# One core, three fused transformer stages: the same steps in another order in three written-out lists

## The reference, cut to what matters

```
# 1: attention, 8 heads of 64; heads 0-3 local (32 keys back), heads 4-7 strided (same position mod 32)
x = softmax(masked(q @ k.T / 8)) @ v
# 2: mixing
theta = x @ w_theta
zr, zi = x * cos(theta), x * sin(theta)
u = x + w_tok_r @ zr + w_tok_i @ zi          # over tokens
x = u + relu(u @ w_ch)
# 3: four attention experts with causal softmax; each token takes the best 2 of 4 gates
logits = x @ w_gate; w = softmax(top 2 of logits)
for e in range(4):
    q, k, v = x @ wq[e], x @ wk[e], x @ wv[e]
    out += gate[e] * (causal_softmax(q @ k.T / 8) @ v @ wo[e])
```

## Time and profile before

| | |
|---|---|
| median of 3 runs | 561.27 us (560.54 to 561.74) |
| the profiled execution, its time | 561.68 us |
| its span | 559.9 us |
| busy: PE, DVE, ACT, POOL | 538.1, 320.1, 236.9, 109.5 us |
| mean granted clock of TensorE | 0.994 |
| share of the chain that ended last: PE, DVE, ACT, POOL | 80%, 7%, 2%, 1% |

### The profile page before, as it was taken

How to read it: one execution, slowest core, us unless ns; L and a number is a source line. 1 busy time by engine, 2 the same in 40 slices (tenths; PEclk the granted TensorE clock), 3 DMA queues, 4 the chain that set the end, 5 groups by cost and what they waited for, 6 DMA issues and landing times.

```text
span 559.9 us, 13648 instructions
## 1 busy us (share of the span) xinstructions
PE 538.1 (96%) x5593; PEld 455.5 (81%) x5593; DVE 320.1 (57%) x795; ACT 236.9 (42%) x599; POOL 109.5 (20%) x123
## 2 busy tenths in 40 slices
...
GB/s 214 177 174 26 52 39 189 136 61 28 2 2 2 37 49 125 88 45 45 2 2 2 19 67 75 96 83 31 21 1 0 20 67 1 1 2 1 1 1 85
DMA packets 79997, 28.97 MB, mean 52 GB/s; under 512 B 75200, under 2 KB 75200, under 8 KB 79936
## 3 DMA queue, kind: packets, MB, share of 16 engines
...
## 4 chain that ended last, share of the span: by engine, by line
PE 80%; DVE 7%; SPq 5%; ACT 2%; issue 2%; DMA 1%; POOL 1%; POOLq 0%; DVEq 0%; ACTq 0%
PE acc L1227 41%; PE wide L1227 16%; PE wide L1326 4%; PE turned L1419 3%; PE turned L1360 2%; SPq L604 2%; PE turned L1461 2%; DVE nmax L982 2%; PE turned L1346 2%; PE turned L1395 2%; PE wide L1380 2%; PE wide L1305 2%; PE turned L1260 1%; DMA raw_v<-in_v 1%; SPq L607 1%
## 5 line engine op out<-in xcount | busy, mean ns | idle before, releaser
L769 POOL TENSOR_TENSOR xu_lo<-xt,xu_hi 128x576 fp32r<-128x576 f32 x15 | 21.0, 1411 | 207.3 <-ACT xu_hi L861 207.3
L759 POOL TENSOR_TENSOR probs<-probs,weight 128x128 f32<-128x128 f32 (+4 forms) x36 | 26.9, 767 | 156.9 <-DVE weight L1036 156.9
L839 ACT ACTIVATE probs<-wide,nmax 128x128 f32<-128x128 f32 (+4 forms) x72 | 39.2, 554 | 36.0 <-DVE nmax L982 35.8
L834 ACT ACTIVATE tiled<-wide,nmax 128x64 f32<-128x64 f32 x176 | 39.2, 330 | 24.0 <-DVE nmax L978 20.2
L1227 PE MATMUL wide<-w_tok_hi,z_hi 128*128 128x288 f32 x216 | 47.5, 301 | 0.0
L1227 PE MATMUL wide<-w_tok_lo,z_hi 128*128 128x288 f32 x216 | 46.3, 295 | 0.0
L1227 PE MATMUL wide<-w_tok_hi,z_lo 128*128 128x288 f32 x216 | 46.3, 295 | 0.0
L850 ACT ACTIVATE pt<-turned 128x384 f32<-128x384 f32 (+1 forms) x32 | 16.5, 516 | 56.5 <-PE turned L1360 56.5
L1227 PE MATMUL acc<-xu_hi,w_ch_hi 128*128 128x288 f32 x128 | 39.3, 307 | 1.0 <-DVE xu_lo L1125 0.9
L1227 PE MATMUL acc<-x_hi,w_qk_hi 128*128 128x288 f32 x128 | 39.7, 310 | 0.0
L982 DVE TENSOR_REDUCE nmax<-wide 128x1 f32<-128x128 f32 (+4 forms) x72 | 33.9, 512 | 8.2 <-PE wide L1331 8.1
...
## 6 DMA issues: line engine op xcount, KB each, us to landing
...
```

Of the source, the lines that this page charges most:

```text
L759: ins = g.tensor_tensor(pr, pr, weight[:, j:j + 1].broadcast_to([P, n]), ALU.mult)
L769: g.tensor_tensor(xu[1][:, p, :], xt[:, p, :], xu[0][:, p, :].bitcast(F32), ALU.subtract)\
L834: e = a.activation(tiled[:, t, hh * W:(hh + 1) * W], wide[slot][:, at0:at0 + W], ACT.Exp, bias=nmax[:, hh, t:t + 1])
L839: e = a.activation(probs[:, hh, to0:to0 + n], wide[slot][:, at0:at0 + n], ACT.Exp, bias=nmax[:, hh, j:j + 1], accum_out=sums[:, hh, j:j + 1])
```

## The change

The steps of the three lists are the same, each as often as before. Their order differs in all three; no other line of the kernel is changed. Cut to the places named later ("-" before, "+" after):

```diff
 PROLOGUE = [
-    ("tail", "s1", 2, 0, 2), ("piece", 0), ("back", "s1", 0, 0), ("turn", "s1", 1, 0), ("scores", "s1", 2, 0),
-    ("max", "s1", 2, 0, 0), ("piece", 1), ("values", "s1", 1, 0), ("max", "s1", 2, 0, 1), ("exp", "s1", 2, 0, 0),
...
+    ("warm", 1, "acc", 1), ("prep", "s1", 2, 0, "acc"), ("max", "s1", 1, 0, 0), ("max", "s1", 1, 0, 1), ("piece", 0),
+    ("piece", 1), ("exp", "s1", 1, 0, 0), ("exp", "s1", 1, 0, 1), ("norm", "s1", 0, 0), ("copied", "s1", 2, 0),
+    ("tail", "s1", 2, 0, 2), ("turn", "s1", 1, 0), ("scores", "s1", 2, 0), ("max", "s1", 2, 0, 0),
+    ("exp", "s1", 2, 0, 0), ("warm", 1, "acc", 1), ("weights", 2), ("back", "s1", 0, 0), ("prep", "s1", 3, 0, "acc"),
...
-    ("done", "theta", 3), ("trig", 1), ("trig", 2), ("products", 1), ("split", 0), ("done", "theta", 4), ("trig", 3),
-    ("split", 1), ("trig", 4), ("wave", 0, 0, 0, 2), ("wave", 0, 1, 0, 2), ("products", 2), ("split", 2),
-    ("wave", 0, 0, 2, 3), ("products", 3), ("wave", 0, 1, 2, 3), ("split", 3), ("products", 4), ("wave", 1, 0),
...
+    ("done", "wtok", 6, "wide"), ("products", 0), ("theta", 4), ("done", "theta", 3), ("trig", 1), ("products", 1),
+    ("split", 0), ("trig", 2), ("done", "theta", 4), ("products", 2), ("split", 1), ("wave", 0, 0, 0, 2),
+    ("wave", 0, 1, 0, 2), ("trig", 3), ("trig", 4), ("split", 2), ("products", 3), ("wave", 0, 0, 2, 3),
+    ("products", 4), ("wave", 0, 1, 2, 3), ("piece", 2), ("piece", 3), ("split", 3), ("wave", 1, 0),
...
-    ("piece", 7), ("piece", 8), ("mix", 3), ("weights", 8),
+    ("mix", 3), ("piece", 8), ("weights", 8),
 BODY = [
-    ("max", "s1", 2, 0, 1), ("done", "v", 4), ("copied", "s1", 3, 0), ("exp", "s1", 2, 0, 1), ("values", "s1", 1, 0),
-    ("back", "s1", 0, 0), ("norm", "s1", 1, 0), ("tail", "s1", 3, 0), ("qk", 0, 0), ("back", "s1", 1, 0),
...
-    ("exp", "s1", 3, 0, 1), ("qk", 2, 1), ("done", "qk", 2, 0), ("done", "qk", 2, 1), ("turn", "s1", 3, 0),
-    ("gate", 0, 5), ("scores", "s3", 0, 0), ("max", "s3", 0, 0, 0), ("qk", 1, 0), ("values", "s1", 3, 0, "turned"),
...
-    ("max", "s3", 0, 1, 1), ("exp", "s3", 0, 1, 0), ("turn", "s3", 0, 0, 1), ("theta", 0, 0, 2),
-    ("norm", "s3", 0, 1, 0), ("xu", 3), ("values", "s3", 0, 0), ("theta", 0, 2, 3), ("theta", 0, 3, 4),
-    ("exp", "s3", 0, 1, 1), ("scores", "s3", 1, 0), ("theta", 1, 0, 2), ("norm", "s3", 0, 1, 1), ("done", "theta", 0),
-    ("max", "s3", 1, 0, 0), ("turn", "s3", 0, 1, 0), ("exp", "s3", 1, 0, 0), ("max", "s3", 1, 0, 1),
...
-    ("products", 0), ("theta", 4, 2, 4), ("turn", "s3", 2, 0, 1), ("done", "theta", 4), ("out", 1),
-    ("values", "s3", 2, 0), ("trig", 1), ("done", "out", 1), ("products", 1), ("trig", 2), ("out", 2),
-    ("done", "out", 2), ("out", 3), ("split", 0), ("done", "out", 3), ("products", 2), ("trig", 3), ("out", 4),
-    ("done", "out", 4), ("split", 1), ("wave", 0), ("products", 3), ("split", 2), ("trig", 4), ("wave", 1),
-    ("products", 4), ("split", 3), ("split", 4), ("wave", 2), ("wave", 3), ("wave", 4), ("mix", 3),
...
+    ("done", "v", 4), ("back", "s1", 0, 0), ("values", "s1", 1, 0), ("norm", "s1", 1, 0), ("qk", 0, 0),
+    ("rank", 0, 5), ("tail", "s1", 3, 0), ("exp", "s1", 2, 0, 1), ("qk", 0, 1), ("done", "qk", 0, 0),
...
+    ("back", "s1", 2, 0), ("qk", 1, 0), ("done", "qk", 2, 1), ("gexp", 0, 5), ("turn", "s1", 3, 0), ("xu", 2),
+    ("gate", 0, 5), ("scores", "s3", 0, 0), ("done", "qk", 1, 0), ("max", "s3", 0, 0, 0), ("max", "s3", 0, 0, 1),
...
+    ("exp", "s3", 0, 1, 0), ("theta", 0, 0, 2), ("turn", "s3", 0, 0, 1), ("norm", "s3", 0, 1, 0),
+    ("exp", "s3", 0, 1, 1), ("theta", 0, 2, 3), ("xu", 3), ("values", "s3", 0, 0), ("norm", "s3", 0, 1, 1),
+    ("scores", "s3", 1, 0), ("max", "s3", 1, 0, 0), ("theta", 0, 3, 4), ("theta", 1, 0, 2), ("done", "theta", 0),
...
+    ("turn", "s3", 1, 0, 0), ("max", "s3", 1, 1, 0), ("turn", "s3", 1, 0, 1), ("theta", 2, 2, 3), ("out", 0),
...
+    ("theta", 3, 0, 2), ("max", "s3", 2, 0, 1), ("exp", "s3", 2, 0, 1), ("norm", "s3", 2, 0, 0), ("done", "out", 0),
+    ("theta", 3, 2, 3), ("values", "s3", 1, 1), ("theta", 3, 3, 4), ("turn", "s3", 2, 0, 0), ("norm", "s3", 2, 0, 1),
+    ("theta", 4, 0, 2), ("trig", 0), ("theta", 4, 2, 4), ("done", "theta", 3), ("turn", "s3", 2, 0, 1), ("trig", 1),
+    ("done", "theta", 4), ("out", 1), ("products", 0), ("values", "s3", 2, 0), ("products", 1), ("trig", 2),
+    ("done", "out", 1), ("out", 2), ("trig", 3), ("products", 2), ("done", "out", 2), ("split", 0), ("trig", 4),
+    ("products", 3), ("out", 3), ("done", "out", 3), ("products", 4), ("out", 4), ("done", "out", 4), ("split", 1),
+    ("wave", 0), ("split", 2), ("wave", 1), ("split", 3), ("split", 4), ("wave", 2), ("wave", 3), ("wave", 4),
 EPILOGUE = [
-    ("scores", "s3", 2, 0), ("turn", "s3", 1, 1, 0), ("max", "s3", 2, 0, 0), ("out", 0), ("gexp", 4, 5),
-    ("gate", 4, 5), ("max", "s3", 2, 0, 1), ("done", "out", 0), ("turn", "s3", 1, 1, 1), ("exp", "s3", 2, 0, 0),
-    ("exp", "s3", 2, 0, 1), ("out", 1), ("done", "out", 1), ("norm", "s3", 2, 0, 0), ("out", 2),
-    ("norm", "s3", 2, 0, 1), ("values", "s3", 1, 1), ("turn", "s3", 2, 0, 0), ("turn", "s3", 2, 0, 1),
-    ("values", "s3", 2, 0), ("out", 3), ("done", "out", 2), ("done", "out", 3), ("out", 4), ("done", "out", 4),
...
+    ("gexp", 4, 5), ("max", "s3", 2, 0, 1), ("gate", 4, 5), ("out", 0), ("out", 1), ("exp", "s3", 2, 0, 1),
+    ("values", "s3", 1, 1), ("norm", "s3", 2, 0, 0), ("norm", "s3", 2, 0, 1), ("done", "out", 0), ("done", "out", 1),
+    ("out", 2), ("out", 3), ("done", "out", 2), ("turn", "s3", 2, 0, 0), ("turn", "s3", 2, 0, 1),
+    ("values", "s3", 2, 0), ("out", 4), ("done", "out", 3), ("done", "out", 4),
```

More of the change, by code:

```diff
@@ L112 @@
[L112 to L116, removed]
@@ L127 @@
-    ("piece", 7), ("piece", 8), ("mix", 3), ("weights", 8),
+    ("warm", 1, "acc", 1), ("max", "s1", 0, 0, 0), ("max", "s1", 0, 0, 1), ("prep", "s1", 1, 0, "acc"),
+    ("exp", "s1", 0, 0, 0), ("warm", 6, "turned", 0), ("exp", "s1", 0, 0, 1), ("copied", "s1", 1, 0),
+    ("tail", "s1", 1, 0, 2), ("turn", "s1", 0, 0), ("scores", "s1", 1, 0), ("values", "s1", 0, 0),
+    ("warm", 1, "acc", 1), ("prep", "s1", 2, 0, "acc"), ("max", "s1", 1, 0, 0), ("max", "s1", 1, 0, 1), ("piece", 0),
+    ("piece", 1), ("exp", "s1", 1, 0, 0), ("exp", "s1", 1, 0, 1), ("norm", "s1", 0, 0), ("copied", "s1", 2, 0),
@@ new lines @@
+    ("tail", "s1", 2, 0, 2), ("turn", "s1", 1, 0), ("scores", "s1", 2, 0), ("max", "s1", 2, 0, 0),
+    ("exp", "s1", 2, 0, 0), ("warm", 1, "acc", 1), ("weights", 2), ("back", "s1", 0, 0), ("prep", "s1", 3, 0, "acc"),
[3 rows of a table added]
+    ("norm", "s1", 2, 0), ("warm", 2, "acc", 1), ("exp", "s1", 3, 0, 0), ("warm", 2, "acc", 1), ("xu", 1),
+    ("back", "s1", 2, 0), ("exp", "s1", 3, 0, 1), ("wtok", 0, "acc"), ("xu", 2), ("turn", "s1", 3, 0),
+    ("done", "wtok", 0, "acc"), ("wtok", 5, "wide"), ("values", "s1", 3, 0, "turned"), ("norm", "s1", 3, 0, "turned"),
@@ L128 @@
+    ("wtok", 4, "turned"), ("done", "wtok", 4, "turned"), ("piece", 6), ("wave", 3, 1), ("wave", 4), ("piece", 7),
+    ("mix", 3), ("piece", 8), ("weights", 8),
 ]
 BODY = [
[L133 to L136, removed]
@@ L159 @@
-    ("max", "s3", 1, 0, 0), ("turn", "s3", 0, 1, 0), ("exp", "s3", 1, 0, 0), ("max", "s3", 1, 0, 1),
-    ("theta", 1, 2, 3), ("turn", "s3", 0, 1, 1), ("exp", "s3", 1, 0, 1), ("theta", 1, 3, 4), ("norm", "s3", 1, 0, 0),
-    ("norm", "s3", 1, 0, 1), ("values", "s3", 0, 1), ("turn", "s3", 1, 0, 0), ("done", "theta", 1),
-    ("scores", "s3", 1, 1), ("turn", "s3", 1, 0, 1), ("max", "s3", 1, 1, 0), ("theta", 2, 0, 2),
-    ("exp", "s3", 1, 1, 0), ("norm", "s3", 1, 1, 0), ("theta", 2, 2, 3), ("max", "s3", 1, 1, 1),
```

50 lines of the change are left out of this document (25 added, 25 removed), and 56 rows, old and new, of tables (BODY, EPILOGUE, PROLOGUE).

## The result

The changed kernel takes 558.04 us (median of 19 runs, 554.42 to 560.92), the kernel before 561.27. The ratio is 0.9939, with a 95% interval from 0.9923 to 0.9956: 0.6% or 3.2 us faster, about half of what was forecast.

What follows compares the result with a forecast made beforehand. PE, busy 96%, bounds the kernel, with DVE pacing it in one body stretch. Bodies -7.2, prologue +0.3 and epilogue +0.5 sum to -6.4, forecasting 555.0 us; range 552.5 to 560.2.

Steps and rivals of the forecast that it cites:

- I find all copies done in time: Body, first part: reordered channel steps, v and prep never wait for the copy that frees their slot.
- the 0.8 being switches between transposes and matmuls that the new order saves: Body, first part: about eight saved switches of 0.1, so turn s1 3 starts only 0.4 later.
- There PE's order is paced by DVE: Body stretch 158.16 to 193.18: DVE, busy 31.1 of 35.0 us, sets the pace of PE's order.
- These 0.4 are the same time as DVE's 1.5, not additional: Body, second part: PE's saved waits around theta 0 (0.25 and 0.17) add nothing to DVE's gain of 1.5.
- the meeting: Body, second part: POOL's xu_lo overlaps DVE's norm 0 1 0, whose three TENSOR_SCALARs take 2.17 instead of 1.06.
- the largest term: Body, second part: exp 0 1 1 ahead of xu 3 keeps POOL's xu_lo off DVE's norm 0 1 0, winning 1.1.
- a longer fall would add about 1: Prologue: if longer PE idling costs clock, about 1 us more; counted only in the upper bound of +1.3.
- PE waits longer instead (3.3, from 1.75): Prologue: scores 3 comes 1.9 earlier but values 2 still waits for raw_v, so PE idles longer before it.
- About 0.5 won: Prologue, from values 2 to theta 0: same steps in another order win about 0.5, spent again later.
- A: Rival, 0.21: xu_lo still hits DVE's norm, or the first part's lead shrinks; bodies gain 1.0 each, 559.1 us.
- C: Rival, 0.11, slower: theta 4 waits for out 0's later copy on ACT, holding PE; up to 565 us.
- B: Rival, 0.11: no effect, DVE keeps PE's old pace and gains reappear as waits at values s3 or epilogue; 561 us.

Runs made afterwards that it cites:

- e6: Kernel before with one step of its body's list moved, exp 0 1 1 ahead of xu 3; 565.13 us, ratio 1.0071.
- e9: Kernel before with the changed body's list, but xu 3 directly behind theta 0 2 3 and ahead of exp 0 1 1; 555.16 us, ratio 0.9892.
- e10: Kernel before with exp 0 1 1 and theta 0 2 3 ahead of xu 3, theta 0 3 4 behind scores s3 1 0; 561.40 us, ratio 0.9997.
- e7: Kernel before with one step of its body's list moved, qk 1 0 ahead of turn s1 3; 563.60 us, ratio 1.0058.

## Why the prediction was right in direction, and where its sum was off

| term | forecast | measured |
|---|---|---|
| bodies | -7.2 | -5.5 |
| prologue | +0.3 | +1.95 |
| epilogue | +0.5 | +0.6 |

**Bodies.** "I find all copies done in time" and the moved waits held. Two steps did not.
- *"the 0.8 being switches between transposes and matmuls that the new order saves"*. The turn was to come 0.4 later; the gate that hangs on it comes 1.1 later (148.86 - 100.82 against 145.79 - 98.87). So of the 1.3 to be saved PE saved 0.6, nearly all of it the wait of the earlier trace rows, and the estimate of eight switches is not in the trace. The maxima come 0.6 earlier instead of 1.1, and this is the larger part of the miss: from the maxima to products 1 the body gains 1.05 of the 1.3 that were forecast.
- *"There PE's order is paced by DVE"* and *"These 0.4 are the same time as DVE's 1.5, not additional"*. As far as e6 and e9 show, the pace was held by both in turn, and DVE's gain passed to PE only in part. In the new order about 0.6 of DVE's 1.05 reach PE, and what the later xu 3 costs PE leaves 0.27 (e9). In the old order e6 and e10 avoid the meeting and gain nothing, but each with a new wait of its own, so what the avoided meeting alone is worth there stays open.

So the mechanism called the largest term happened on DVE and POOL as worked out and carries 0.27 of the second body's 1.7; qk 1 0 ahead of the turn, with its copy moved along, carries 0.6. The remaining 0.8 lies at least in part in PE's order between the maxima and products 1: there PE no longer waits between the two turns of pair 0 (0.25), nor 0.3 for DVE's norm ahead of turn s3 1 1 0. That was read from the two traces; no run isolated it. The third body's further 0.5 was in no term of the sum: that the bodies come to 5.5 and not to 5.0 is luck. The parts also do not simply add: e6, e7 and e10 show that moves taken out of the new order cost 1.2, 0.9 and nothing in the old one.

**Prologue.** The risk was foreseen ("a longer fall would add about 1"), but as a bound and not in the sum. It came, with 6.8 us at 1.2 GHz in place of 3.4 in both profiled executions of the new list, and cost 1.5. Its stated cause did not: *"PE waits longer instead (3.3, from 1.75)"* is not in the trace, where values 2 waits for no load and PE idles 1.73 with no releaser, earlier, inside scores 3. Why the fall is longer stays open. "About 0.5 won" from there to theta 0 is hardly there: the changed kernel's 10.89, less some 3.2 for 6.5 us at half clock (an estimate by the 1.65 above), is 7.7, against the old list's 7.8. The +1.95 is the difference of two single executions, in a part that scatters by up to 3.8 us between profiles of one list.

**Epilogue.** As forecast in kind and size. Out 0 and out 1 are copied together behind exp 2 0 1, out 2 waits for the slot, and out 4 waits for DVE's two copies (the earlier trace rows before):

```profile
543.46 1.08 ACT L873 ACTIVATE o_sb<-acc 128x512 f32<-128x512 f32 x2
```

```profile
544.20 0.47 PE L1232 MATMUL acc<-w_o_hi,xu_hi 128*128 128x512 f32 x1 [0.23 <-ACT o_sb L873]
...
552.08 0.42 PE L1232 MATMUL acc<-w_o_hi,xu_hi 128*64 128x512 f32 x1 [0.77 <-DVE xu_hi L1072]
```

**Rivals.** A gave nearly the measured time (559.1 for 558.04) and for another reason: the meeting that it keeps is gone, and the bodies gain 1.8 on average and not 1.0. That the time lies nearer to A's than to the forecast's is luck. What A shares with the result is "the first part's lead shrinks". C did not come: no wait ahead of theta 3 or theta 4 appears among PE's waits of the second body. B, that DVE's gain reappears as a wait, is seen in part in e6 and e10 for the old order.
